# Splitting the queries and keys over the whole pair, with the exponential last in ScalarE's slot

## The reference

```python
scores = scale * np.matmul(q, k.transpose(0, 1, 3, 2))          # attention
kth = np.partition(scores, -32, axis=-1)[..., -32:-31]
scores = np.where(scores >= kth, scores, -1e9)                  # top 32 of each row
attn = softmax(scores); x = attn @ v                            # heads side by side
gate = sigmoid(causal 5-tap convolution of x over tokens)
x = (gate * (x @ w_val)) @ w_out
mixed = real(fft(fft(x, tokens), features)); u = x + mixed      # token and feature mixing
un = layernorm(u)
out = u + relu(un @ w_ch1) @ w_ch2                              # 512 -> 2048 -> 512
```

## Time and profile before

| | us |
|---|---|
| median of 3 runs (lowest, highest) | 1212.93 (1212.51, 1215.17) |
| the profiled execution's own time | 1214.56 |
| its span, first to last instruction | 1212.8 |
| TensorE matmul busy | 1049.4 (87%) |
| VectorE busy | 884.3 (73%) |
| ScalarE busy | 621.3 (51%) |
| GpSimd busy | 406.9 (34%) |
| mean granted TensorE clock | 0.926 of full |

### The profile page before, as it was taken

How to read it: one execution, slowest core, us unless ns; L and a number is a source line. 1 busy time by engine, 2 the same in 40 slices (tenths; PEclk the granted TensorE clock), 3 DMA queues, 4 the chain that set the end, 5 groups by cost and what they waited for, 6 DMA issues and landing times.

```text
span 1212.8 us, 19844 instructions
## 1 busy us (share of the span) xinstructions
PE 1049.4 (87%) x6608; PEld 841.9 (69%) x6608; DVE 884.3 (73%) x1898; ACT 621.3 (51%) x1253; POOL 406.9 (34%) x704
## 2 busy tenths in 40 slices
PE   3776565789798989989798989999798999998998
PEld 2554454666587878866587878775587888648887
DVE  6999999996996978696996978696996970330000
ACT  3786766644565655554565655454565653012221
POOL 2444533142443332233433332322443322133221
PEclk9886756889898999999898999999898999998999
DMA  8566455021355856321355846321365655206974
GB/s 256 163 202 203 140 187 188 11 74 35 102 209 193 282 192 198 134 75 46 111 217 192 270 178 213 123 70 45 126 226 202 226 179 204 108 1 237 351 277 162
DMA packets 81188, 200.37 MB, mean 165 GB/s; under 512 B 8384, under 2 KB 26560, under 8 KB 81088
## 3 DMA queue, kind: packets, MB, share of 16 engines
q1 hardware_dynamic: 81088, 199.11, 48.2%
HBM read 177.58 MB, written 21.50 MB: 164 GB/s over the span
## 4 chain that ended last, share of the span: by engine, by line
PE 56%; issue 14%; DVE 12%; POOL 10%; ACT 5%; DMA 1%; SPq 1%; DVEq 0%; ACTq 0%; POOLq 0%
PE p_m L567 15%; PE p_m L553 15%; PE p_m L461 14%; DVE rest L742 5%; PE p_t L434 4%; PE p_t L450 4%; PE p_s L421 4%; DVE top L748 3%; ACT prob L630 2%; POOL k_lo L876 2%; POOL bias L884 1%; POOL hid_lo L949 1%; POOL w_st L901 1%; POOL bias L885 1%; DMA u<-w_ch 1%
## 5 line engine op out<-in xcount | busy, mean ns | idle before, releaser
L748 DVE MAX8 top<-rest 128x8 f32<-128x576 f32 x432 | 304.7, 747 | 0.0
L949 POOL TENSOR_TENSOR hid_lo<-hid,hid_hi 128x256 fp32r<-128x256 f32 (+1 forms) x128 | 107.0, 836 | 325.8 <-ACT hid_hi L692 325.8
L742 DVE MATCH_REPLACE8 rest<-top,rest 128x576 f32<-128x576 f32 x288 | 211.7, 743 | 0.0
L553 PE MATMUL p_m<-un_hi,w_st 128*128 128x320 f32 (+1 forms) x1024 | 172.9, 313 | 44.6 <-POOL un_lo L940 25.3
L567 PE MATMUL p_m<-w_st,hid_hi 128*128 128x512 f32 x640 | 206.3, 404 | 0.2 <-POOL hid_lo L949 0.2
L553 PEld LDWEIGHTS p_m<-un_hi,w_st 128*128 128x128 f32 x1024 | 149.6, 198 | 55.5 <-POOL un_lo L940 26.2
L630 ACT ACTIVATE prob<-s_sb,bias 128x576 f32<-128x576 f32 x144 | 111.1, 772 | 105.0 <-POOL bias L885 104.6
L623 ACT ACTIVATE s_sb<-p_s 128x576 f32<-128x576 f32 x144 | 93.1, 646 | 136.3 <-PE p_s L421 136.2
L434 PE MATMUL p_t<-id_sb,prob 128*128 128x128 f32 x720 | 122.1, 306 | 34.4 <-ACT or_sb L652 34.0
L421 PE MATMUL p_s<-k_hi,q_st 128*128 128x512 f32 (+1 forms) x320 | 118.2, 372 | 33.2 <-POOL k_lo L876 19.5
L450 PE MATMUL p_t<-pT,v_sb 128*64 128x128 f32 (+1 forms) x1600 | 106.9, 285 | 43.5 <-ACT pT L643 23.4
(11 more groups left out here) (78 smaller groups left out, 1602.9 us busy)
## 6 DMA issues: line engine op xcount, KB each, us to landing
w_st<-w_split SPq DMA_DIRECT2D x256, 512.0 KB, 4.4
w_split<-w_st SPq DMA_DIRECT2D x32, 512.0 KB, 3.0
q_raw<-qT SPq DMA_DIRECT2D x64, 144.0 KB, 3.4
k_raw<-kT SPq DMA_DIRECT2D x64, 144.0 KB, 3.4
u<-w_ch SPq DMA_DIRECT2D x32, 256.0 KB, 3.6
v_sb<-v SPq DMA_DIRECT2D x16, 256.0 KB, 3.5
wslot<-w_val SPq DMA_DIRECT2D x4, 1024.0 KB, 5.3
wslot<-w_out SPq DMA_DIRECT2D x4, 1024.0 KB, 5.3
```

What stands on the lines that cost most here:

```text
L553: mm = pe.matmul(mbank(HIDDEN_BANK[g], n), w1_st[i % NB1][:, w, k, :], x[:, k, at:at + n], start=part + k == 0, stop=part + k == KC + 1)
L742: dve.match_replace(rest[tt % 2][:, :], top[tt % 4][:, 8 * n - 8:8 * n], src[:, :], LOWEST).then_inc(s_chain, 1)
L748: found = dve.max(top[tt % 4][:, 8 * n:8 * n + 8], rest[tt % 2][:, :])
L949: pool.tensor_tensor(hid_lo[i % 2][:, 0:WIDTH[g]], hid[:, 0:WIDTH[g]], hid_hi[i % 2][:, 0:WIDTH[g]].bitcast(F32), ALU.subtract).then_inc(m ...
```

## The change

Five edits, all in the order of work and in buffers; the arithmetic is the same.

1. The split queries and keys get two buffers per head (`q_st`, `k_hi`, `k_lo`, indexed by the pair's parity). The raw ones become one buffer for both heads, so loads of head 1 wait for the low parts of head 0 and the reverse; the very first load of head 1 uses the buffer `z`.
2. The splits of the next pair are spread over the pair. ScalarE makes the high queries in tiles 0 (head 0) and 4 (head 1), the high keys in tiles 1 and 5, last in its slot. GpSimd makes head 0's low parts in tile 2, last in its slot; VectorE makes head 1's in tile 6. The loads are issued in tiles 7 (head 0, for the pair after the next) and 3 (head 1), and in slot 0 for head 0 of the second pair.
3. ScalarE's exponential moves behind all steps of its slot.
4. GpSimd's biases move behind all steps of its slot.
5. The first transposes of the normalised rows (`trn` 0 and 1) come before `seq` 2 and `proj` 4, and the normalisations before them move with them. In slots: 52 gets `proj` 3, `trn` 0; 53 gets `seq` 2, `trn` 1; 54 gets `proj` 4, `ch0` 0 (before: `proj` 3 | `seq` 2, `trn` 0, `proj` 4 | `trn` 1, `ch0` 0).

```diff
+STEPS += [("seq", 0), ("proj", 0), ("proj", 1), ("seq", 1), ("proj", 2), ("proj", 3), ("trn", 0), ("seq", 2), ("trn", 1),
+          ("proj", 4)]
-NORM_AT = {("proj", 2): 0, ("seq", 2): 1, ("ch0", 1): 2, ("ch0", 4): 3, ("ch0", 7): 4}
+NORM_AT = {("proj", 1): 0, ("proj", 2): 1, ("ch0", 1): 2, ("ch0", 4): 3, ("ch0", 7): 4}
+LOAD = {7: 0, 3: 1}
+HIGH_Q, HIGH_K, LOW = {0: 0, 4: 1}, {1: 0, 5: 1}, {2: 0, 6: 1}
@@ scalar: the head of a pair's splits @@
+                def high_queries(p, h):
                     act.wait_ge(s_qk_in[h], 64 * (p + 1))
-                    if p:
-                        act.wait_ge(s_qk, TILES * p)
-                    else:
+                    if p >= 2:
+                        act.wait_ge(s_qk, TILES * (p - 1))
+                    elif p == 0:
                         act.wait_ge(s_zero, FILLS)
@@ scalar: the slot @@
                         store_pT(s - TRANSPOSE)
-                    if split_due(s) is not None:
-                        split_high(split_due(s), 0)
-                        split_high(split_due(s), 1)
-                    if due(s, EXPONENT):
-                        exponent(s - EXPONENT)
                     if part_due(s) is not None:
                         split_weights(part_due(s))
...
                     for x in plan[s][1:]:
                         step(*x)
+                    if due(s, EXPONENT):
+                        exponent(s - EXPONENT)
+                    p, i = divmod(s, TILES)
+                    if p + 1 < ALL_PAIRS and i in HIGH_Q:
+                        high_queries(p + 1, HIGH_Q[i])
+                    if p + 1 < ALL_PAIRS and i in HIGH_K:
+                        high_keys(p + 1, HIGH_K[i])
@@ vector: the slot @@
-                    if split_due(s) is not None:
-                        split_low(split_due(s))
+                    p, i = divmod(s, TILES)
+                    if p + 1 < ALL_PAIRS and LOW.get(i) == 1:
+                        split_low(p + 1)
@@ gpsimd: the slot @@
-                    if split_due(s) is not None:
-                        split_low(split_due(s))
-                    if due(s, EXPONENT):
-                        biases(s - EXPONENT)
                     if part_due(s) is not None:
                         split_weights(part_due(s))
                     for x in plan[s][0:1]:
...
                     for x in plan[s][1:]:
                         step(*x)
+                    if due(s, EXPONENT):
+                        biases(s - EXPONENT)
+                    p, i = divmod(s, TILES)
+                    if p + 1 < ALL_PAIRS and LOW.get(i) == 0:
+                        split_low(p + 1)
@@ sync: the slot @@
-                    if i == 1 and p + 1 < ALL_PAIRS:
-                        load_qk(p + 1, 0)
-                        load_qk(p + 1, 1)
+                    if s == 0:
+                        load_qk(1, 0)
+                    ahead = p + 2 - LOAD.get(i, 0)
+                    if i in LOAD and ahead < ALL_PAIRS:
+                        load_qk(ahead, LOAD[i])
```

More of the change, by code:

```diff
@@ L21 @@
 NS = 6
-FILLS = 17
+FILLS = 19
 TOPK = 32
@@ L133, in build @@
         power = sb("power", [P, 1])
[L135 to L139, removed]
+        q_raw = sb("q_raw", [P, S])
+        k_raw = sb("k_raw", [P, S])
+        q_st = [[sb(f"q_st{h}{i}", [P, SP], F32R) for i in range(2)] for h in range(2)]
+        k_hi = [[sb(f"k_hi{h}{i}", [P, S], F32R) for i in range(2)] for h in range(2)]
+        k_lo = [[sb(f"k_lo{h}{i}", [P, S], F32R) for i in range(2)] for h in range(2)]
         v_sb = [sb(f"v_sb{i}", [P, NCH, P]) for i in range(2)]
@@ L257, in due, with raw @@
             return 0 <= s - lag < ALL_TILES
+        def raw(p, h):
+            if p == 0 and h == 1:
+                flat = z[:, :, :].rearrange("p c n -> p (c n)")
+                return flat[:, 0:S], flat[:, S:2 * S]
+            return q_raw[:, :], k_raw[:, :]
         def unit_due(s):
@@ L298, in load_qk @@
                 def load_qk(p, h):
-                    if p:
-                        sp.wait_ge(s_lo[h], (2 + h) * p)
+                    if h:
+                        if p:
+                            sp.wait_ge(s_lo[0], 2 * (p + 1))
+                    elif p == 1:
+                        sp.wait_ge(s_lo[0], 2)
+                    elif p:
+                        sp.wait_ge(s_lo[1], 3 * p)
+                    q, k = raw(p, h)
                     b, p = divmod(p, PAIRS)
@@ L303, in load_qk @@
                         rows = slice(D * half, D * half + D)
-                        sp.dma_start(q_raw[h][rows, :], qT[b, 2 * p + h]).then_inc(s_qk_in[h], 16)
-                        sp.dma_start(k_raw[h][rows, :], kT[b, 2 * p + h]).then_inc(s_qk_in[h], 16)
+                        sp.dma_start(q[rows, :], qT[b, 2 * p + h]).then_inc(s_qk_in[h], 16)
+                        sp.dma_start(k[rows, :], kT[b, 2 * p + h]).then_inc(s_qk_in[h], 16)
                 def load_v(p):
@@ L418, in scores @@
                     for k0, k1 in ((0, BANK), (BANK, S)):
-                        parts = [(h, k) for h in heads for k in (k_hi[h], k_lo[h])]
+                        parts = [(h, k[h][p % 2]) for h in heads for k in (k_hi, k_lo)]
                         for n, (h, k) in enumerate(parts):
-                            mm = pe.matmul(p_s[:, k0:k1], q_st[h][:, cols], k[:, k0:k1],
+                            mm = pe.matmul(p_s[:, k0:k1], q_st[h][p % 2][:, cols], k[:, k0:k1],
                                            start=n == 0, stop=n == len(parts) - 1)
@@ L692, in step @@
                         act.activation(hid_hi[i % 2][:, 0:WIDTH[g]], bank, ACT.Relu).then_inc(m_hev, 1)
-                split_high(0, 0)
-                split_high(0, 1)
+                for h in range(2):
+                    high_queries(0, h)
+                    high_keys(0, h)
                 for s in plan:
@@ L873, in split_low @@
                     pool.wait_ge(s_hi, 5 * p + 2)
-                    pool.tensor_tensor(q_st[0][0:D, 0:S], q_raw[0][0:D, :], q_st[0][0:D, 0:S].bitcast(F32),
+                    q, k, high = q_st[0][p % 2], k_lo[0][p % 2], k_hi[0][p % 2]
+                    q_in, k_in = raw(p, 0)
+                    pool.tensor_tensor(q[0:D, 0:S], q_in[0:D, :], q[0:D, 0:S].bitcast(F32),
                                        ALU.subtract).then_inc(s_lo[0], 1)
-                    pool.tensor_tensor(k_lo[0][:, :], k_raw[0][:, :], k_hi[0][:, :].bitcast(F32),
+                    pool.tensor_tensor(k[:, :], k_in, high[:, :].bitcast(F32),
                                        ALU.subtract).then_inc(s_lo[0], 1)
```

25 lines of the change are left out of this document (13 added, 12 removed).

## The result

The changed kernel takes 1295.45 us (median of 4 runs, 1292.77 to 1299.45) against 1213.55 (4 runs, 1212.51 to 1215.17) beside it: 1.068 times the time, 95% interval 1.064 to 1.071. Slower, as forecast, but by 82 us where the forecast had 38, and outside its range. The profiled execution spans 1297.7 us; at 1299.45 us it is the slowest of the four, 4 us over the median.

A forecast was written before the change was run, and what follows sets the result against it. VectorE bounds the first batch's attention, TensorE with gaps the rest; terms 30 + 5 + 1 + 14 - 9 - 3 = +38 on 1214.6 give 1252.6, or 1251.0 us as median; range 1207 to 1275.

The forecast's parts named there:

- first batch, start and ring (to slot 43): First batch: late start plus ring-bound slots 5 to 33, together +30 us; bounds +11 and +42 (all attends slow).
- values, three times: Slots 43 to 47 and their like: 2.78 us gap goes, but biases wait behind the fold; +5 us, bounds -10, +12.
- MLP, first rows: Slots 55 to 65 and their like: TensorE loses 13.6 us instead of 9.0, +4.6 per batch, +14 in all.
- MLP, other rows: Later MLP slots, wider steps: losses of 2.9 replace 3.13 + 2.9 us; -3.1 per batch, -9 in all.
- last batch: Last batch, without exponentials: the 3.65 us wait shrinks to 0.9 us; -3 us.
- the ring: Exponential, score copy, transposed copy, step, GpSimd's part, biases, exponential: 5.46 us a slot without an attend, 6.14 with one.
- The rival by which the ring does not bind: Whole kernel: ring does not bind and TensorE's gaps go, about 1160 us; chance 0.15.
- The contention rival: GpSimd's biases slowed by VectorE's shared SBUF port, some 20 slots a batch: +25 us, 1276; chance 0.05.
- First term: Start: slot 1's copy waits behind high queries for transfers, +10.7 us; bounds 5 and 12, about 5.5 by the skill.
- Second term: Rest of slots 5 to 33: the ring takes 177 us, +19 us, with 6 added for low clock and feature matmuls.
- Fourth term: Projections and transposes: 7.19 us gap goes, biases wait for GpSimd's deviation; +0.3 per batch, +1; bounds -9, +4 per batch.
- What was to show it: Signs: slot 1's copy at 23 to 25 us, VectorE gaps for score copies, ScalarE waiting for biases, attends for transposed copies.

The follow-up runs named there:

- run 1: Changed kernel with GpSimd's biases back at the start of its slot, exponential still last: 1169.5 us, ratio 0.963.
- run 6: Kernel before with only the late exponential and late biases, old buffers and splits: 1309.1 us, ratio 1.079.
- run 4: Changed kernel with the second pair's splits put later in the first pair, to where their transfers have landed: 1295.1 us, ratio 1.067.
- run 11: Changed kernel with biases and exponential early in all slots and later splits in the first pair: 1162.9 us, ratio 0.958.
- run 5: Changed kernel with 92 added TensorE matmuls that nothing reads, in slots 14 to 35: 1287.1 us, ratio 1.059.
- run 3: Changed kernel with eight `top` buffers instead of four, biases and exponential still last: 1292.9 us, ratio 1.065.
- Run 9: Changed kernel with biases early only in slots carrying values or projections, late in all others: 1239.7 us, ratio 1.022.
- run 8: Changed kernel with biases early, exponential early up to slot 35 and late after, later splits in the first pair: 1155.3 us, ratio 0.952.

## Why the prediction failed in size

Forecast against measured, read off the slots' starts (slots 43, 48, 54, 66, 79 and their like):

| term | forecast | measured |
|---|---|---|
| first batch, start and ring (to slot 43) | +30 | +55.7 |
| values, three times | +5 | +0.8 +4.6 +4.5 = +9.9 |
| projections and transposes | +1 | +9.5 +10.1 +9.2 = +28.8 |
| MLP, first rows | +14 | +1.3 +1.8 -1.8 = +1.3 |
| MLP, other rows | -9 | -2.2 -2.4 +0.0 = -4.6 |
| last batch | -3 | 84.9 - 91.0 = -6.1 |
| sum on the profiled executions | +38 | +84.9 |

**The mechanism was right.** Biases last on GpSimd and the exponential last on ScalarE close the ring that the forecast lists link by link; run 1 opens it and 126 us go, run 6 closes it on the old buffers. Whether it needs both late places is not shown. The rival by which the ring does not bind gave 1160: that is what the kernel does once it is opened (1169.5). The contention rival fell: the two bias instructions average 0.24 and 0.32 us in the changed kernel against 0.29 and 0.33 before.

**First term, the start: right in size, wrong as a term of a sum.** The slots show 11.6 us at slot 1 and 10.1 at slot 5 (forecast 10.7), but run 4 takes it away and gains nothing, while run 11 gains 9.5. With the late biases other waits of slots 4 to 12 take it up; where VectorE works without a gap it passes through to the end. (The forecast's two lower figures are a little off: landings after 2 and 2.3 us give 5.8 and 6.2 by its own reckoning, not 5 and 5.5.)

**Second term: the price of the attend link was mis-sized.** The step that failed is "attend start until the bias 2.58". It came from a row at the full clock. From the exponential of slot 4 to that of slot 33 (36.62 to 233.86) 197.2 us pass instead of 177. Of the 20 us, nine slots whose attend takes 2.40 us hold 11.7 (1.30 each). Three slots with an attend at the full clock hold 5.5, because eight matmuls for the features stand ahead of it (one of them, in slot 8; the transposed copy is ready at 58.4):

```profile
56.24 5.10 PE L481 MATMUL p_m<-gv,gate 128*128 128x512 f32 x8
...
61.27 1.31 PE L470 MATMUL p_t<-pT,v_sb 128*64 128x128 f32 x20
```

Slots without an attend hold the other 3. For clock and feature matmuls together the forecast had added 6 us, and these took 17. It had kept "all attends slow" for the far bound, though before already 8 of 16 attends in that stretch were slow. What I had not asked is what a ring does to the clock; run 5 measures what the clock gives back, 7.3 us of the 11.7. VectorE was 7 us in hand as counted when slot 34 came (its search is 45.9 us late, the copy 52.3), but at slot 43, where the table is read, the copy is still 55.7 late. The wait over `top`, which I had missed, is worth 2.6 us at most (run 3).

**Fourth term: "zero within my reach" was wrong by 28 us**; 9.6 us a batch lie outside its bound of +4. The deviation was named as the link, but only one attend was followed. The chain in slots 85 and 86 of the changed kernel:

```profile
620.86 3.70 PE L481 MATMUL p_m<-wslot,gv 128*128 128x512 f32 x8
...
624.70 0.43 DVE L832 TENSOR_TENSOR u<-p_m,pm 128x257 f32<-128x257 f32 x1 [6.26 <-PE p_m L481]
...
625.49 0.69 DVE L835 BATCH_NORM_STATS2 stats<-u 128x6 f32<-128x512 f32 x1
...
626.49 0.22 POOL L957 TENSOR_SCALAR rstd<-mv 128x1 f32<-128x1 f32 x1 [3.19 <-DVE mv L837]
626.80 0.57 POOL L959 TENSOR_TENSOR rstd<-rstd,power 128x1 f32<-128x1 f32 x1
627.45 0.24 POOL L916 TENSOR_SCALAR bias<-top 128x1 f32<-128x1 f32 x1
...
628.12 0.78 ACT L654 ACTIVATE prob<-s_sb,bias 128x576 f32<-128x576 f32 x1 [6.55 <-POOL bias L917]
...
630.43 0.63 ACT L647 ACTIVATE s_sb<-p_s 128x576 f32<-128x576 f32 x1
630.96 0.69 ACT L667 ACTIVATE pT<-p_t 128x640 f32<-128x640 f32 x1
...
631.70 1.49 PE L470 MATMUL p_t<-pT,v_sb 128*64 128x128 f32 x20 [2.50 <-ACT pT L667]
```

TensorE's projection, VectorE's sum and statistics, GpSimd's deviation and biases, ScalarE's exponential and copies stand one behind another, 10.8 us until the attend. In run 1 the same attend follows its projection after 8.3 us. Run 9 puts it right and gets 56 us back with the values.

**The MLP's terms erred the other way together.** The first rows lost 13 us less than forecast and the other rows gained 4 less: the gaps that went paid for the ring there. That the ring binds in the MLP as well is shown by run 1, where these two stages are 11 and 4 us shorter in each of the first two batches than as changed. Against before, run 1's are 10 and 6 us shorter: for the first rows the forecast had the vanishing gaps about right (9.0) and the ring's losses too high (13.6 against 11).

**What was to show it** held in the main: slot 1's copy behind a transfer, the exponential's wait for biases the longest on ScalarE, the attends of slots 57 and 59 waiting for the transposed copy, the attend of slot 80 behind fold and biases. VectorE had its gaps from 40 us on, but biases ended them (21.0 us between 30 and 220 us) and not score copies. None of these observations could tell 38 from 82 us.

## What to carry to other kernels

Where an order closes a ring over several engines, price each link at the clock that the ring itself will leave: here the 1.31 us row turned into a 2.40 us one in nine slots of the first batch. Walk every stage slot by slot with the longest chain ahead of the moved instruction, not one example of it. And put small instructions that others wait for (two of 0.3 us here) ahead of steps that wait for third engines: the late exponential alone gains 39 us (3 where the two buffers and edit 5 are in already), and with the biases late as well, behind other engines' work, all is lost.

## What the runs showed of the hardware

Work that nothing reads made the kernel 8.4 us faster: 92 matmuls of 128x512 raised the granted clock of a 156 us stretch from 0.62 to 0.96 and brought the attends from 2.07 to 1.20 us on average. Where VectorE sets the pace the low clock seems to cost nothing: the kernel before has 0.69 in the same stretch and run 8 has 0.68, with 8 and 9 of 16 attends slow, and VectorE is busy for 155.3 of the 156 us in both. No run raised the clock there.
